# Last stage of an attention, routing and mixing kernel: theta ahead of the mix by three tiles, angles by one, and the first weight splits in front

## The reference

```python
theta = x @ w_theta                      # x: (2, 768, 512), w_theta: (512, 512)
cos_t, sin_t = (np.cos(theta), np.sin(theta))
zr = x * cos_t
zi = x * sin_t
yr = np.einsum('ts,bsd->btd', w_tok_r, zr)   # w_tok_r, w_tok_i: (768, 768)
yi = np.einsum('ts,bsd->btd', w_tok_i, zi)
u = x + yr + yi
return (u + np.maximum(u @ w_ch, 0.0)).astype(np.float32)
```

## Time and profile before

| | |
|---|---|
| runs | 575.3, 575.65, 577.1 us, median 575.65 |
| profiled execution | 577.11 us |
| its span, first to last instruction | 575.1 us |
| TensorE busy | 497.2 us (86%) |
| VectorE busy | 282.9 us (49%) |
| ScalarE busy | 197.7 us (34%) |
| mean granted TensorE clock | 0.95 of 2.4 GHz |
| last stage | from the first scaled tile at 379.2 us to the end |

### The profile page before, as it was taken

One profiled execution on the slowest core, in us unless ns is written; L12 is line 12 of the kernel. 1 busy time (PEld: TensorE's weight loads), 2 busy tenths in 40 slices (PEclk: granted clock), 3 DMA queues, 4 the chain that ended last, 5 costly groups with the idle time before them and its releaser, 6 DMA issues.

```text
span 575.1 us, 9081 instructions
## 1 busy us (share of the span) xinstructions
PE 497.2 (86%) x3216; PEld 419.2 (73%) x3217; DVE 282.9 (49%) x631; ACT 197.7 (34%) x411; POOL 116.3 (20%) x116
## 2 busy tenths in 40 slices
PE   0899999920299999999999999947999999999987
PEld 0577777710299989889889889835788878888866
DVE  5567887543221233251441441138888776555143
ACT  1578887602011323141331331133544322222010
POOL 3966775015200202020220200062000000000000
PEclk9999999965599999999999999967999999999999
DMA  7735455764341284655694731053000000000012
GB/s 270 268 117 173 142 180 176 318 265 159 128 171 48 84 337 150 269 200 226 259 400 156 294 125 36 18 145 93 0 1 0 2 1 19 18 19 19 19 38 92
DMA packets 22177, 78.16 MB, mean 136 GB/s; under 512 B 2944, under 2 KB 3200, under 8 KB 18048
## 3 DMA queue, kind: packets, MB, share of 16 engines
q0 software_dynamic: 8032, 46.67, 20.8%
q1 hardware_dynamic: 11520, 26.89, 14.0%
q10 hardware_dynamic: 2592, 4.20, 2.2%
HBM read 62.01 MB, written 15.73 MB: 135 GB/s over the span
## 4 chain that ended last, share of the span: by engine, by line
PE 64%; issue 19%; DVE 9%; DMA 3%; ACT 3%; DVEq 1%; ACTq 0%; POOLq 0%; SPq 0%; POOL 0%
PE ps L1136 34%; PE ps L1161 10%; PE ps L1010 5%; PE ps L1068 5%; PE ps L1052 4%; PE ps L1032 3%; DMA w_sb<-in_w_experts 2%; PE ps L1222 1%; DVE w_lo L889 1%; PE ps L1147 1%; PE ps L1184 1%; DVE z L912 1%; DMA x_tok<-slots,slot 1%; DVE near L687 1%; ACT w_hi L587 1%
## 5 line engine op out<-in xcount | busy, mean ns | idle before, releaser
L1161 PEld LDWEIGHTS ps<-xT,w_sb 128*128 128x128 f32 x1024 | 118.2, 194 | 5.5 <-issue 3.1
L1161 PE MATMUL ps<-xT,w_sb 128*128 128x128 f32 x1024 | 118.7, 277 | 3.3 <-DMA w_sb<-in_w_experts 2.3
L880 DVE SCALAR_TENSOR_TENSOR hT_lo<-ps,hT_hi 128x512 fp32r<-128x512 f32 x32 | 21.8, 688 | 98.2 <-ACT hT_hi L574 98.0
L889 DVE TENSOR_TENSOR w_lo<-w_sb,w_hi 128x1024 fp32r<-128x1024 f32 x32 | 37.0, 1219 | 47.4 <-ACT w_hi L587 47.4
L1136 PE MATMUL ps<-w_hi,hT_hi 128*128 128x512 f32 x128 | 51.4, 402 | 2.2 <-DVE hT_lo L880 2.2
L528 ACT ACTIVATE prob<-raw,row_min 128x256 f32<-128x256 f32 (+1 forms) x96 | 46.2, 484 | 14.4 <-DVE row_min L749 13.3
L467 POOL DMA_DIRECT2D w_sb<-in_w_experts x32 | 17.3, 543 | 164.5 <-PE ps L1136 141.6
L1136 PE MATMUL ps<-w_hi,hT_lo 128*128 128x512 f32 x128 | 50.0, 391 | 0.0
L1136 PE MATMUL ps<-w_lo,hT_hi 128*128 128x512 f32 x128 | 49.9, 390 | 0.0
L574 ACT ACTIVATE hT_hi<-ps 128x512 fp32r<-128x512 f32 x32 | 19.0, 595 | 85.0 <-PE ps L1161 85.0
L578 ACT COPY yout<-ps 128x512 f32<-128x512 f32 x16 | 9.4, 586 | 89.8 <-PE ps L1136 89.8
(11 more groups left out here) (177 smaller groups left out, 976.5 us busy)
## 6 DMA issues: line engine op xcount, KB each, us to landing
w_sb<-in_w_experts POOLq DMA_DIRECT2D x32, 1024.0 KB, 9.6
v_sb<-in_vx SPq DMA_DIRECT2D x8, 640.0 KB, 5.0
slots<-zero SPq DMA_DIRECT2D x20, 256.0 KB, 5.5
xin<-slots SPq DMA_DIRECT2D x17, 256.0 KB, 2.7
slots<-yout ACTq DMA_DIRECT2D x16, 256.0 KB, 2.5
k_raw<-in_kx SPq DMA_DIRECT2D x8, 432.0 KB, 6.1
q_raw<-in_q SPq DMA_DIRECT2D x8, 384.0 KB, 6.5
out_x<-o_sb SPq DMA_DIRECT2D x12, 256.0 KB, 2.0
```

The lines of the kernel that those rows point to most:

```text
L880: dve.scalar_tensor_tensor(hT_lo[:, part, :], ps[:, 1 + half, :].rearrange("p (c q) -> p c q", c=4), 0.0, hT_hi[:, part, :].bitcast(F32), ...
L889: dve.tensor_tensor(quarter(w_lo, par, q), quarter(w_sb, par, q), w2_hi_quarter(q).bitcast(F32), ALU.subtract).then_inc(s_w2_lo, 1)
L1161: last = pe.matmul(ps[:, 1 + half, f * P:(f + 1) * P], w_sb[:, par, c // 2, j:j + P], xT[:, c, :], start=(c == 0), stop=(c == DC - 1))
```

## The change

Theta runs three tiles ahead of the mix. theta(0) goes into bank 5 and theta(1) into bank 4, which the first mix reaches last; the other thetas stay in bank 7. From theta(3) on theta waits for the reduce_angle before; the first three don't. The mix waits at i == 4 of its first tile until both early angles are read. On VectorE reduce_angle goes a tile ahead of rotate. weights_high(0), weights_low(0) go to the front of their engines' work, the other slices go behind rotate, one tile further ahead, and weigh runs three tiles ahead. The thresholds of the waits that guard banks 6 and 7 move by one tile with it.

```diff
--- before.py
+++ after.py
@@ -118,6 +118,11 @@
 def channel_bank(n):
 
     return 7 if n < QT else n % QT
+
+
+def theta_bank(n):
+
+    return (5, 4)[n] if n < 2 else 7
 
 
 def wait(eng, sem, value):
@@ -630,22 +635,23 @@
                     act.copy(wch_hi[:], wch[:]).then_inc(s_w_hi, 1)
 
 
+            weights_high(0)
             act.activation(ang_a[:, 0:1], half_pi[:, 0:1], ACT.Sin)
             x_high(0)
-            weights_high(0)
+            x_high(1)
+            weights_high(1)
+            x_high(2)
             for s in range(-2, NT):
                 m, n = s + 2, s - QT
                 if n >= 0:
                     u_high(n)
-                if m + 1 < NT:
-                    x_high(m + 1)
-                if 2 <= m < QT:
-                    weights_high(m + 1)
+                if 0 < m < NT - 2:
+                    x_high(m + 2)
                 if m < NT:
                     rotation(m)
                     z_high(m)
-                if m < 2:
-                    weights_high(m + 1)
+                if m < QT - 1:
+                    weights_high(m + 2)
             for n in range(QT, NT):
                 u_high(n)
 
@@ -910,8 +916,8 @@
                 wait(dve, s_e_zl, n)
                 for m in range(2):
                     dve.tensor_tensor(z[:, m, :], x_tok[:, n, :], trig[:, m, :], ALU.mult).then_inc(s_e_z, 1)
-                if n + 2 < NT:
-                    weigh(n + 2)
+                if n + 3 < NT:
+                    weigh(n + 3)
                 dve.wait_ge(s_e_z, 2 * (n + 1))
                 dve.wait_ge(s_e_zh, n + 1)
                 low(z_lo[:, n % 2, :, :], z[:], z_hi[:, n % 2, :, :]).then_inc(s_e_zl, 1)
@@ -927,7 +933,7 @@
 
             def reduce_angle(n):
                 dve.wait_ge(s_e_th, n + 1)
-                th = ps[:, 7, :]
+                th = ps[:, theta_bank(n), :]
                 wait(dve, s_e_trig, 2 * (n - 1))
                 then(dve.tensor_scalar(ang_k[:], th, float(1 / (2 * np.pi)), MAGIC, ALU.mult, ALU.add))
                 then(dve.tensor_scalar(ang_k[:], ang_k[:], MAGIC, None, ALU.subtract))
@@ -960,27 +966,30 @@
 
             dve.wait_ge(s_w_hi, 1)
             low(wth_lo[:], wth[:], wth_hi[:]).then_inc(s_w_lo, 1)
+            weights_low(0)
             weigh(0)
+            x_low(0)
             weigh(1)
-            x_low(0)
-            weights_low(0)
+            x_low(1)
+            weights_low(1)
+            weigh(2)
+            reduce_angle(0)
+            x_low(2)
             for s in range(-2, NT):
                 m, n = s + 2, s - QT
                 if n >= 0:
                     u_low(n)
-                if m < NT:
-                    reduce_angle(m)
                 if m + 1 < NT:
-                    x_low(m + 1)
+                    reduce_angle(m + 1)
+                if 0 < m < NT - 2:
+                    x_low(m + 2)
                 if s == QT - 1:
                     for i in range(QT):
                         add_y(i)
-                if 2 <= m < QT:
-                    weights_low(m + 1)
                 if m < NT:
                     rotate(m)
-                if m < 2:
-                    weights_low(m + 1)
+                if m < QT - 1:
+                    weights_low(m + 2)
                 if n >= 0:
                     finish(n)
             add_y(QT)
@@ -1179,18 +1188,19 @@
             def turn_x2(n):
                 pe.wait_ge(s_x2, n + 1)
                 wait(pe, s_e_xl, n)
-                wait(pe, s_e_ul, n - QT - 2)
+                wait(pe, s_e_ul, n - QT - 3)
                 for c in range(DC):
                     last = pe.transpose(ps[:, 6, c * P:(c + 1) * P], x_tok[:, n, c * P:(c + 1) * P], ident)
                 last.then_inc(s_e_tx, 1)
 
             def theta(n):
                 pe.wait_ge(s_e_xl, n + 1)
-                wait(pe, s_e_rr, n)
-                wait(pe, s_e_o, n - QT - 2)
+                if n > 2:
+                    pe.wait_ge(s_e_rr, n)
+                wait(pe, s_e_o, n - QT - 3)
                 if n == 0:
                     pe.wait_ge(s_w_lo, 1)
-                exact(ps[:, 7, :], [((x2T_hi[:, n % 2, c, :], x2T_lo[:, n % 2, c, :]), (wth_hi[:, c, :], wth_lo[:, c, :]))
+                exact(ps[:, theta_bank(n), :], [((x2T_hi[:, n % 2, c, :], x2T_lo[:, n % 2, c, :]), (wth_hi[:, c, :], wth_lo[:, c, :]))
                                     for c in range(DC)], True, True).then_inc(s_e_th, 1)
 
             def mix(n, part):
@@ -1202,6 +1212,8 @@
                     if b == 0:
                         pe.wait_ge(s_w_lo, n + 2)
                 for i in range(QT):
+                    if part == 0 and n == 0 and i == 4:
+                        pe.wait_ge(s_e_rr, 2)
                     if part == 0 and n == QT:
                         pe.wait_ge(s_e_u, i + 1)
                     q = slice(i * P, (i + 1) * P)
@@ -1214,7 +1226,7 @@
             def turn_u(n):
                 pe.wait_ge(s_e_u, n + 1)
                 if n < QT:
-                    pe.wait_ge(s_e_xl, min(n + QT + 3, NT))
+                    pe.wait_ge(s_e_xl, min(n + QT + 4, NT))
                 wait(pe, s_e_ul, n if n <= QT else n - 1)
                 if n > QT:
                     pe.wait_ge(s_e_o, QT)
@@ -1225,7 +1237,7 @@
             def channels(n):
                 pe.wait_ge(s_e_ul, n + 1)
                 if n < QT:
-                    pe.wait_ge(s_e_rr, min(n + QT + 3, NT))
+                    pe.wait_ge(s_e_rr, min(n + QT + 4, NT))
                     wait(pe, s_e_o, n)
                 if n == 0:
                     pe.wait_ge(s_w_lo, QT + 2)
@@ -1234,17 +1246,20 @@
                        for c in range(DC)], True, True).then_inc(s_e_v, 1)
 
             turn_x2(0)
-            for n in range(2):
-                theta(n)
-                turn_x2(n + 1)
+            theta(0)
+            turn_x2(1)
+            turn_x2(2)
+            theta(1)
+            theta(2)
+            turn_x2(3)
             for s in range(NT):
                 mix(s, 0)
                 if s >= QT:
                     turn_u(s - QT)
-                if s + 2 < NT:
-                    theta(s + 2)
                 if s + 3 < NT:
-                    turn_x2(s + 3)
+                    theta(s + 3)
+                if s + 4 < NT:
+                    turn_x2(s + 4)
                 mix(s, 1)
                 if s >= QT:
                     channels(s - QT)
```

## The result

| | before | changed |
|---|---|---|
| median of 7 runs | 575.66 us (573.26 to 578.46) | 583.18 us (579.77 to 585.21) |
| ratio, with its 95% interval | | 1.0121 (1.009 to 1.0151) |
| profiled execution, span | 577.11, 575.1 us | 581.77, 579.7 us |
| mean granted clock | 0.950 | 0.941 |

The change makes the kernel slower by 1.2%, which is 7.0 us (5.2 to 8.7). In these two profiled executions the last stage began 1.9 us earlier in the changed kernel (376.10 and 374.22 us for the start of wth_lo on VectorE), by the scatter of what comes before (two further traces of the changed kernel have this start at 375.03 and 376.90). So from here on a position in **R us** is counted from the start of wth_lo. From there to the last instruction it is 199.0 us before and 205.5 us after: **+6.5 us**.

What follows compares the result with a forecast made beforehand. The last stage's opening was taken as bound by a loop TensorE, ScalarE, VectorE, TensorE, the rest by TensorE. The mix's lateness, less theta done ahead and a removed wait, gave 575.65 + 5.9 = 581.5 us, range 578.8 to 584.0.

Steps and rivals of the forecast that it cites:

- Steps 1 and 2: Start of the last stage: front weight splits make weigh(0) 0.85 us late, of which 0.24 us is left at theta(0).
- Step 3: Opening: x_low(1) comes 2.4 us earlier, uncollected, as turn_x2(2) ahead of theta(1) waits for weigh(2) until 393.20.
- rival (b): Three tiles ahead keep TensorE fed and spare banks bring a gain: 6.5 us faster, 569.1 us; chance 0.06.
- Step 4: Transposes of tile 2 at low clock, 0.9 us to theta(1), which starts at 394.1, 1.5 us late.
- Step 5: VectorE's opening: reduce_angle(0) late, rotate(0) behind reduce_angle(1), so the first mix starts 8.6 us late.
- step 7: Between the first mix's halves: theta(3) waits for x_low(3), behind weights_low(2) and reduce_angle(2), and starts at 413.2.
- Step 6: Spare banks 5 and 4 alone give nothing; the mix's added wait at i == 4 costs nothing.
- Step 8: mix(0,1) 9.2 us late, less 3.15 us for the theta done ahead and an old 0.2 us wait: +5.9 us.
- Step 9: Behind the opening: VectorE's about 10 us a tile stays covered by TensorE's 11.4; batch change and drain keep their order.
- Rival (a): Opening: the clock stays at 2.4 GHz through theta(1); +3.9, 579.5 us; chance 0.13.
- Rival (d): Opening: the low clock covers all of mix(0,0) and theta(3); +9.7, 585.3 us; chance 0.09.
- Rival (c): No change, 575.65 us: theta done ahead makes up the mix's lateness, needing idle TensorE time behind 418 us; chance 0.04.

Runs made afterwards that it cites:

- e2: Changed kernel with rotate(0) put ahead of reduce_angle(1) on VectorE, for tile 0 alone; ratio 1.0114 to the kernel before.
- e9: Kernel before with only the spare banks 5 and 4 for theta(0) and theta(1) and the mix's wait at i == 4; executed once, 577.23 us.
- e1: Changed kernel with weigh(2) put ahead of weights_low(1) on VectorE; ratio 1.0038 to the kernel before.
- e7: Changed kernel with 17 matmuls of no use behind turn_x2(1), filling TensorE's hole in the opening; ratio 1.0108 to the kernel before.
- e10: Changed kernel with tile 1 transposed ahead of theta(0), early splits and weighs beside theta(0), rotate(0) ahead of reduce_angle(1), theta still three ahead; ratio 1.002 to before.
- e8: Changed kernel with five matmuls of no use in the drain, ahead of turn_u(6); ratio 1.0102 to the kernel before.

## Why the prediction was right

The forecast was 581.5 us in 578.8 to 584.0; the median is 583.18, and the direction and the chain are as predicted. That the total came so close is in part luck: the opening costs 0.7 us less than forecast, and 1.4 us in the drain, which the prediction did not have, more than make up for it. By its own steps:

- Steps 1 and 2: weigh(0) 0.85 us late, theta(0) 0.24 us late. Both as measured (R 3.95 for 3.10, 7.00 for 6.76).
- Step 3, on which rival (b) hung: turn_x2(2) at 393.20 - 376.10 = R 17.1, measured R 16.8, held by weigh(2). The 0.3 us is theta(0), whose clock rose a little earlier, 4.83 us for 5.09.
- Step 4: 0.9 us from transposes to theta(1), measured 0.76; theta(1) 1.1 us late and not 1.5.
- Step 5: the mix 8.6 us late, measured 7.7. The term that was too large is theta(1) at the low clock, 4.86 us to its reduce_angle and not 5.29. **The words around this step were wrong**: "Only behind reduce_angle(1) comes rotate(0) ... This is the dear part." e2 removes just this, and mix(0, 1) comes no earlier. The dear part is the sum of VectorE's work up to x_low(3), reduce_angle(2) included, ahead of the second half of the first mix, which step 7 had right.
- Step 6: right in e9 as to the bank; its wait costs nothing in the changed order, but it does in the old one.
- Step 7: theta(3) at R 37.1, measured 36.5. Both sides of that step are close together in the changed kernel: x_low(3) ends at 410.37 (R 36.2), and theta(3) comes 0.4 us later without a wait, behind a mix whose first twelve matmuls ran at the low clock. In e1, e2, e7 and e10 it does wait for x_low(3).
- Step 8: +5.9 us, measured +5.2 in the opening (mix(0, 1) 8.5 us late, less 3.15 and 0.2).
- Step 9: no wait was added behind the opening, as said. **The term that was missing** is 1.4 us of low clock in the drain. I had checked the orders there and not the clock. 5.2 + 1.4 = 6.6, and the end moved 6.5.

Rival (a), the clock kept through theta(1), did not occur; e7 brings it about and is worth 1.1 us where I had 2.0. Rival (d) did not occur: the clock was back after twelve matmuls of the mix. Rival (c) fails on the full TensorE from 413.84 to 470.43. Rival (b) was named with its deciding point, theta(1) before 391 or after 393 (R 14.9 or 16.9): it started at R 17.6. That point was itself not enough: e10 has theta(1) at R 12.8 and is still no faster than the kernel before (1.002). The Trainium skill's advice to rotate matmul groups through banks ("Perfetto Trace Analysis", section "Matmuls") brought nothing in e9, where theta(1) waited for x_low(1) and not for a bank: it started at R 16.3 for 16.5.

## What to carry to other kernels

Running a producer one tile further ahead can move work of every engine in its loop in front of the consumer's first tiles, as it did here on VectorE; add that work up on the slowest engine of the loop before counting a spare buffer as a gain. Here an opening reordered so that one early theta filled a wait gained 0.7%, and the same opening with theta a tile further ahead throughout lost it again. When an order written by hand is changed, trace for each wait not only who signals it but what stands in front of the signaller in its own queue: weigh(2), 0.48 us long, held TensorE because it stood behind a weight split that waited for ScalarE.

## What the runs showed of the hardware that I had not expected

- Short waits can cost more than their length. After 2.03 us of idle time in e9 and 4.37 in e10 the matmuls first ran as at the full clock and slowed only after some of them (in e10 from the fourth, 0.52 and then 0.63 us shown); in the changed kernel the clock fell behind a wait of 1.38 and one of 0.80 us in the drain. In e9 this made 0.8 us of delay into 1.8. The Trainium skill tells of a kernel whose small idle times between groups of matmuls, frequent enough, made the clock oscillate ("TensorE: Matmul & The Clock Gate", section "A second HAM failure mode: psum-queue depth-cycling"). These traces agree in that the clock fell behind such gaps, from 1.00 to 0.66 over the 4.4 us of channels(6), but in eight other kernels the same two waits did not bring it down.
- The same point of the program kept its clock from trace to trace: three traces of the changed kernel agree in channels(6) (4.6 us), and so do two of e8 (3.2); e10, with other timing, has 4.8. That speaks against pure chance, but each of the other kernels was traced once, so chance isn't excluded, and which kernels lose the clock there I could not derive.
- Work of no use can be worth its time: five matmuls in an idle stretch came with an end 1.4 us earlier in two traces of two, and seventeen in the opening with mix(0, 1) 1.1 us earlier in one.
